# The second keys' grams between the two sums of P, two unread products for three, and the weights rounded in six parts

## The chip, the cores and the metric

The kernel runs on one core of a Trainium2 chip. The metric is the device time of one execution in microseconds (us). TensorE multiplies matrices, VectorE (DVE) and ScalarE (ACT) do elementwise work, GpSimd (POOL) does too, and SyncE (SP) issues most transfers. TensorE's weight loads are listed as an engine of their own (PEld).

## The reference

Three stages in a row. The first is a delta rule over 768 time steps for 4 batches and 8 heads of dimension 48. The second is a linear layer pair with a product. The third is a soft mixture with 8 experts of 4 slots each.

```python
# 1, for every t
y[:, :, t] = einsum('bhd,bhde->bhe', q[:, :, t], state)
v_old = einsum('bhde,bhd->bhe', state, kt)          # kt = k / (|k| + 1e-6)
state = state + bt[:, :, :, None] * einsum('bhd,bhe->bhde', kt, vt - v_old)
# 2, x is y as 3072 tokens of 384
h = (x @ w1) * (x @ w2) @ w3                        # d_ff 1024
x = h @ w_out
# 3, phi is 384 x 32
logits = x @ phi
d = softmax of logits over the tokens; c = softmax over the slots
slot_input = d.T @ x
slot_out[e] = relu(slot_input[e] @ e1[e]) @ e2[e]
out = c @ slot_out
```

## The kernel before

The 768 time steps are cut into 24 tiles of 32 steps (`g` = 0 to 23), 4 tiles to an iteration (`n` = 0 to 5). A tile holds 4 batches times 32 steps in the 128 partitions.

For an iteration the inner products of all keys of a tile with each other and with the queries ("grams", `gram_products`, L1087) are made on TensorE. Out of them a triangular system is solved by elementwise steps (`set_up`, `set_up_rest`, then 30 steps of a product and a sum), scaled (`scale`, L831 and L834) and turned (`turn_back`, L840) into `TM`. For the first iteration VectorE does the 30 steps itself (L819, L820). For each later iteration GpSimd does them (L485, L486), while the tiles of the iteration before are worked on. `scale(n + 1)` on VectorE waits for GpSimd's last step and stands, in VectorE's order, in front of a product a * b of tile `4n + 3` (`ab_mul`, L745).

For each tile TensorE then multiplies keys and queries with the state (`key_query_state`, L1103), solves (`solve_rows`, L1118, which waits for `TM`), updates the state (L1137), makes y (`y_step`, L1152), turns it (`x_turn`, L1164), and multiplies the turned x with w1 and w2 (`up`). Tile 0 does so in plain float32 (L1180). All later tiles use three products of high and low halves (L1201), for which ScalarE rounds the weights to `whi` (`w_high`, L598) and VectorE makes the rest `wlo` (`w_low`, L848). The product a * b is turned by `ab_turn` (L1219).

Ahead of the tiles stands a prologue. P = w3 @ w_out @ phi is made in two steps: w_out with phi (L1273), a sum of its partial results (`add_parts`, L1265), then w3 with that (L1284), and a second sum (L1265). ScalarE copies between them (`part_out`, L602, and the copies to `wp_sb`, L608, and `P_sb`, L614).

Behind the second sum TensorE makes the grams of the second iteration, waits for P, and runs three 128 x 512 products that nobody reads, each after a semaphore (L1299 to L1301). In front of the first grams stand `FILLERS` tiny products (L1255) that nobody reads either. A float32 product is two weight loads and two matmul instructions, so 47 fillers show as x94 and three products as x6.

Every engine runs its list in order. SP issues in this order: first keys, phi, the transposed w_out, the two halves of the transposed w3, the second keys (eight transfers of 192 KB, 1.5 MB), values, w1, w2.

ScalarE's order in the prologue and in tiles 0 and 1 is: first sums, `key_merge` for tile 1, second sums and P, the four pairs of gram copies, `w_high(0)`, Z of tile 0, x of tile 0 (`y_out`), the turned x of tile 0 (`x_high`), `w_high(1)`, then a of tile 0.

## Time and profile before

| what | value |
|---|---|
| three runs | 493.09, 494.03, 495.74 us; median 494.03 |
| the profiled execution | 495.12 us, its span 493.4 us |
| busy share of the span | TensorE 91%, VectorE 50%, ScalarE 46%, GpSimd 38% |
| mean granted TensorE clock | 0.969 of full speed |
| chain of work that ended last | TensorE 71%, VectorE 10%, GpSimd 8%, DMA 5% |

A row of a timeline gives start and duration in us, engine, source line, operation, tiles, shape and count, and in brackets the engine's idle time before it with what ended it. "issue" there means that nothing which the profile shows was waited for. [...]

### The profile page before, as it was taken

The page shows a single profiled execution, that of the slowest core. Times are in us where ns is not written, and L with a number is a line of the kernel's source. Part 1 is how long each engine was busy: PE and PEld are TensorE (multiplying, and loading weights), DVE is VectorE, ACT ScalarE, POOL GpSimd, SP SyncE. Part 2 cuts the span into 40 slices and gives each one's busy share as a digit, 9 for nine tenths or more (in the row PEclk, how much of TensorE's full clock was granted, in tenths as well). Part 3 has the DMA queues.
Part 4 walks back from the last instruction along what each step waited for, and adds up shares of the span by engine and source line. Part 5 has one row for each costly group of instructions (what it writes and reads, how often), then busy time and mean ns, then how long its engine had stood idle before and what let it go on. Part 6 is the DMA issues. An engine that isn't in the chain of part 4 may idle for free.

```text
span 493.4 us, 21402 instructions
## 1 busy us (share of the span) xinstructions
PE 450.5 (91%) x9729; PEld 323.8 (66%) x9729; DVE 244.4 (50%) x499; ACT 227.9 (46%) x408; POOL 188.4 (38%) x329
## 2 busy tenths in 40 slices
PE   4674899998999999999999999999999999999982
PEld 3243467776777777687677777676787777754442
DVE  3899586355553647346284345644362422144123
ACT  1313455553645555655455565554564464224112
POOL 1001499811588403886028880178830000000000
PEclk9965999999999999999999999999999999999997
DMA  8999305320004400054000641000080094699949
GB/s 205 383 243 336 87 3 112 104 49 5 3 19 113 132 5 3 3 131 130 4 3 4 125 116 24 3 4 4 3 337 9 3 356 160 241 418 425 420 169 372
DMA packets 21002, 64.96 MB, mean 132 GB/s; under 512 B 2352, under 2 KB 3760, under 8 KB 20016
## 3 DMA queue, kind: packets, MB, share of 16 engines
q1 hardware_dynamic: 20208, 62.71, 38.7%
q8 instruction: 77, 1.26, 1.1%
q10 hardware_dynamic: 704, 0.89, 0.7%
q14 instruction: 13, 0.11, 0.1%
HBM read 58.87 MB, written 4.72 MB: 129 GB/s over the span
## 4 chain that ended last, share of the span: by engine, by line
PE 71%; DVE 10%; POOL 8%; DMA 5%; issue 3%; SPq 1%; ACT 0%; DVEq 0%; POOLq 0%
PE pA L1201 19%; PE pB L1201 18%; PE pKY L1103 4%; POOL prep_slab L486 4%; DMA step_slab<-e_dram 4%; POOL prod_p L485 4%; PE pD L1137 3%; PE pKY L1152 3%; PE pKY L1118 3%; PE pT L1219 3%; PE pG L1219 3%; PE pD L1227 2%; DVE prep_slab L820 2%; DVE prod_p L819 2%; DMA arena<-kq_dram 2%
## 5 line engine op out<-in xcount | busy, mean ns | idle before, releaser
L485 POOL TENSOR_TENSOR prod_p<-prep_slab 128x30 f32<-128x30 f32 (+9 forms) x150 | 75.4, 502 | 42.4 <-DVE prep_slab L812 31.5
L745 DVE TENSOR_TENSOR arena<-a_sb,pB 128x512 f32<-128x512 f32 x41 | 28.1, 686 | 120.3 <-PE pB L1201 120.2
L486 POOL TENSOR_TENSOR prep_slab<-prep_slab,prod_p 128x30 f32<-128x30 f32 (+9 forms) x150 | 82.4, 549 | 11.8
L524 ACT ACTIVATE step_slab<-pKY 32x384 f32<-32x384 f32 x92 | 44.3, 482 | 32.8 <-PE pKY L1152 31.1
L1201 PE MATMUL pB<-whi,xhi 128*128 128x512 f32 x135 | 55.8, 414 | 0.0
L1201 PE MATMUL pB<-whi,xlo 128*128 128x512 f32 x135 | 53.2, 394 | 0.0
L1201 PE MATMUL pB<-wlo,xhi 128*128 128x512 f32 x135 | 53.2, 394 | 0.0
L1201 PE MATMUL pA<-whi,xhi 128*128 128x512 f32 x135 | 51.4, 436 | 0.0
L1201 PE MATMUL pA<-wlo,xhi 128*128 128x512 f32 x135 | 47.0, 399 | 0.0
L1201 PE MATMUL pA<-whi,xlo 128*128 128x512 f32 x135 | 46.1, 397 | 0.0
L466 POOL TENSOR_TENSOR arena<-arena,nrm 128x1152 f32<-128x1152 f32 (+1 forms) x11 | 21.1, 1914 | 45.7 <-DVE prep_slab L834 45.0
L552 ACT ACTIVATE a_sb<-pA 128x512 f32<-128x512 f32 x47 | 28.1, 598 | 15.7 <-PE pA L1201 14.8
L478 POOL TENSOR_SCALAR_AFFINE_SELECT prep_slab<-prep_slab 128x1024 f32<-128x1024 f32 x5 | 6.3, 1265 | 74.3 <-DVE sys_s L785 74.3
L556 ACT ACTIVATE arena<-pG 128x512 f32<-128x512 f32 x24 | 14.4, 599 | 39.3 <-PE pG L1219 39.3
L516 ACT ACTIVATE step_slab<-pKY 128x768 f32<-128x768 f32 (+1 forms) x24 | 19.2, 799 | 22.3 <-PE pKY L1118 22.3
L1201 PEld LDWEIGHTS pB<-whi,xhi 128*128 128x128 f32 x135 | 25.3, 187 | 6.1
L1201 PEld LDWEIGHTS pB<-whi,xlo 128*128 128x128 f32 x135 | 25.4, 188 | 5.8
L1201 PEld LDWEIGHTS pA<-whi,xlo 128*128 128x128 f32 x135 | 25.4, 188 | 5.6
L556 ACT ACTIVATE arena<-pT 128x512 f32<-128x512 f32 x24 | 14.3, 598 | 31.6 <-PE pT L1219 31.5
L1201 PEld LDWEIGHTS pB<-wlo,xhi 128*128 128x128 f32 x135 | 25.4, 188 | 4.8
L1201 PEld LDWEIGHTS pA<-wlo,xhi 128*128 128x128 f32 x135 | 25.4, 188 | 4.7
L542 ACT ACTIVATE step_slab<-arena 48x512 f32<-48x512 f32 x46 | 26.4, 620 | 0.4
(284 smaller groups left out, 889.1 us busy)
## 6 DMA issues: line engine op xcount, KB each, us to landing
arena<-e_dram SPq DMA_DIRECT2D x7, 1536.0 KB, 14.6
arena<-kq_dram SPq DMA_DIRECT2D x44, 192.0 KB, 5.6
late_w<-e_dram SPq DMA_DIRECT2D x4, 1536.0 KB, 10.7
arena<-kv_dram SPq DMA_DIRECT2D x6, 768.0 KB, 5.2
arena<-kv_dram SPq DMA_DIRECT2D x24, 192.0 KB, 5.9
arena<-w3t_dram SPq DMA_DIRECT2D x2, 2048.0 KB, 19.2
arena<-w_dram SPq DMA_DIRECT2D x1, 4096.0 KB, 13.9
out_dram<-late_w SPq DMA_DIRECT2D x6, 576.0 KB, 5.4
```

Of the source, the lines that this page charges most:

```text
L466: nc.gpsimd.tensor_tensor(v, v, nr, ALU.mult).then_inc(vp_done, 1)
L485: link(nc.gpsimd.tensor_tensor(pv, a, x, ALU.mult))
L486: link(nc.gpsimd.tensor_tensor(dst, dst, pv, ALU.add))
L516: nc.scalar.activation(Z[:, banks], pKY[:, banks, 0:DM], ACT.Copy).then_inc(z_done, 1)
L524: nc.scalar.activation(xs[quad(b), :], pKY[quad(quarter(g, b) ^ 1), bank(g, b), 0:DM], ACT.Copy).then_inc(y_done, 1)
L542: nc.scalar.activation(KM[rows_, :, 1 - x], src[:, :, x], ACT.Copy).then_inc(km_done, 1)
L552: nc.scalar.activation(a_sb[:], up_bank(t, half, 0), ACT.Copy).then_inc(a_done, 1)
L556: nc.scalar.activation(ABT[:, s, half * 4:half * 4 + 4].rearrange("p c t -> p (c t)"), (pT, pG)[half][:], ACT.Copy).then_inc(abt_done, 1)
L745: nc.vector.tensor_tensor(ab_tile(s, p)[:, half * HF:(half + 1) * HF], a_sb[:], up_bank(t, half, 1), ALU.mult).then_inc(ab_done, 1)
L1103: last = mm(pKY[o:o + 64, b % 2, h * D:h * D + D], KM[r:r + D, b // 2 * H + h].rearrange("p x c -> p (x c)"), ST[r:r + D, b // 2, h * D:h ...
L1201: last = mm(up_bank(t, half, w), lhs[:, c * 128:(c + 1) * 128], rhs[:, w, c, fc], start=(k == 0), stop=(k == 3 * KC - 1))
L1219: last = nc.tensor.transpose((pT, pG)[half][:, c * 128:(c + 1) * 128], ab_tile(s, p)[:, f0:f0 + 128], ident[:])
```

## The change

The eight transfers of the second keys are issued ahead of the two halves of w3. On TensorE the grams of the second iteration move from behind the second sum to between the first sum and the wait for its copy; on ScalarE their copies move in front of the second `part_out` pair. One of the three unread products (the one behind the second half of the scaling) is dropped, and one filler is added. `w_high` rounds a third of a weight at a time, and its six calls are spread over tiles 0 and 1; `w_low` waits for three of them.

```diff
-FILLERS = 47
+FILLERS = 48
...
+            reload_kq(1, 1)
             load_w3t(0)
             load_w3t(1)
-            reload_kq(1, 1)
             load_kv(0, 0)
...
-            def w_high(i):
+            def w_high(i, c):
                 act.wait_ge(w12_in[i], 16)
-                nc.scalar.activation(whi[:, i], w_raw[i], ACT.Copy).then_inc(whi_done, 1)
+                nc.scalar.activation(whi[:, i, c], w_raw[i][:, c], ACT.Copy).then_inc(whi_done, 1)
...
+            for i in range(STEPS):
+                gram_out(1, i, first_gram[1][i])
+                pt_copy(1, i)
             part_out(2, 128)
             part_out(3, 128)
             act.wait_ge(p_ps, 1)
             nc.scalar.activation(P_sb[:].rearrange("p a b -> p (a b)"), pY[:, 0:FC * NS], ACT.Copy).then_inc(p_done, 1)
-            for i in range(STEPS):
-                gram_out(1, i, first_gram[1][i])
-                pt_copy(1, i)
-            w_high(0)
...
                         z_out(g)
+                        w_high(0, 0)
                         y_out(g)
+                        w_high(0, 1)
                         continue
...
                     x_high(t)
                     if g == 1:
-                        w_high(1)
+                        w_high(0, 2)
+                        w_high(1, 0)
...
                     a_out(t, 0)
+                    if g == 1:
+                        w_high(1, 1)
+                        w_high(1, 2)
...
-                dve.wait_ge(whi_done, i + 1)
+                dve.wait_ge(whi_done, KC * (i + 1))
...
             add_parts(pK, 32 * KC, wp_ps)
+            pe.wait_ge(gs_done, STEPS)
+            pe.wait_ge(pt_raw, STEPS)
+            for r in range(2):
+                pe.wait_ge(kq_in[1][r], keys_landed(1, 0))
+            apart(pe, pe_passed)
+            for pair in range(2):
+                gram_products(1, pair, first_gram[1][2 * pair:2 * pair + 2])
             pe.wait_ge(wp_done, 1)
...
             add_parts(pY, 128, p_ps)
 
-            pe.wait_ge(gs_done, STEPS)
-            pe.wait_ge(pt_raw, STEPS)
-            for r in range(2):
-                pe.wait_ge(kq_in[1][r], keys_landed(1, 0))
-            apart(pe, pe_passed)
-            for pair in range(2):
-                gram_products(1, pair, first_gram[1][2 * pair:2 * pair + 2])
             pe.wait_ge(p_done, 1)
 
-            for sem_, i in ((r_done, 1), (x_link, 1), (x_link, 2)):
+            for sem_, i in ((r_done, 1), (x_link, 1)):
```

## Rows read from the trace of the kernel before

**Rows 1.** The page's slices: granted TensorE clock in tenths, 40 equal slices

```profile
PEclk9965999999999999999999999999999999999997
```

**Rows 2.** The chain that ended last, in order of time: start us, us, what

```profile
45.89 2.03 DVE TM L840
...
48.40 1.17 DVE prep_slab L777
...
55.19 1.24 DVE prep_slab L812
...
98.94 1.24 DVE prep_slab L831
100.31 0.69 DVE arena L745
101.04 0.66 PE pG L1219 x4
```

**Rows 3.** Timeline of TensorE, prologue, tile 0 and start of tile 4

```profile
16.56 3.19 PE L1273 MATMUL pKY<-arena,phi_sb 128*32 128x512 f32 x12 [3.52 <-DMA arena<-wot_dram]
...
22.96 3.41 PE L1284 MATMUL pKY<-arena,wp_sb 128*32 128x512 f32 x16 [0.47 <-ACT wp_sb L608]
28.61 2.89 PE L1284 MATMUL pKY<-arena,wp_sb 128*32 128x512 f32 x16 [2.24 <-DMA arena<-w3t_dram]
32.20 3.62 PE L1265 MATMUL pKY<-same,TM 128*128 128x32 f32 x16 [0.70 <-ACT TM L602]
...
46.22 4.65 PE L1301 MATMUL pKY<-Macc,ident 128*128 128x512 f32 x6
50.80 0.88 PE L1118 MATMUL pKY<-step_slab,TM 32*32 32x48 f32 x64
...
55.00 2.84 PE L1180 MATMUL pA<-late_w,cN 128*128 128x512 f32 x6 [0.58 <-ACT cN L546]
...
99.80 1.15 PE L1103 MATMUL pKY<-step_slab 48*64 48x48 f32 x64
```

**Rows 4.** Waits, 0 to 120 us: in total, times, longest

```profile
DVE prep_slab L831 <- POOL prep_slab L486: 4.2, 1, 4.2
```

**Rows 5.** Timeline of VectorE, end of the first system

```profile
43.91 0.56 DVE L724 TENSOR_TENSOR step_slab<-arena,nrm 128x384 f32<-128x384 f32 x1
...
45.64 0.22 DVE L834 TENSOR_TENSOR prep_slab<-sys_s 128x32 f32<-128x32 f32 x1
```

**Rows 6.** Waits of TensorE, 33 to 102 us

```profile
PE pB L1087 <- issue: 6.4, 1, 6.4
```

**Rows 7.** Windows: busy us (instructions) by engine, granted clock, DMA share, GB/s

```profile
16.00:24.00 8.00, 6.18 (x36) 3.04 (x40) 7.11 (x28) 2.62 (x4) 0.00 (x0) 0.91 1.05 387
26.00:34.00 8.00, 5.07 (x29) 2.31 (x25) 7.35 (x20) 1.19 (x2) 0.00 (x0) 0.71 1.06 231
...
46.00:49.00 3.00, 3.00 (x24) 1.28 (x9) 3.00 (x3) 2.64 (x5) 2.12 (x1) 0.50 1.04 407
50.00:52.00 2.00, 1.69 (x67) 0.79 (x65) 1.84 (x5) 0.98 (x2) 1.26 (x1) 1.00 1.01 197
```

**Rows 8.** Timeline of ScalarE, tile 0

```profile
47.97 2.76 ACT L598 ACTIVATE whi<-late_w 128x3072 fp32r<-128x3072 f32 x1
51.75 0.49 ACT L516 ACTIVATE step_slab<-pKY 128x384 f32<-128x384 f32 x1 [1.02 <-PE pKY L1118]
53.33 0.49 ACT L521 ACTIVATE step_slab<-pKY 128x384 f32<-128x384 f32 x1 [1.08 <-PE pKY L1152]
54.45 0.49 ACT L546 ACTIVATE cN<-pT 128x384 f32<-128x384 f32 x1 [0.64 <-PE pT L1164]
```

**Rows 9.** Timeline of GpSimd, three neighbouring steps of the second system

```profile
67.14 0.91 POOL L485 TENSOR_TENSOR prod_p<-prep_slab 128x210 f32<-128x210 f32 x1
68.12 2.62 POOL L486 TENSOR_TENSOR prep_slab<-prep_slab,prod_p 128x210 f32<-128x210 f32 x1
70.82 0.59 POOL L485 TENSOR_TENSOR prod_p<-prep_slab 128x220 f32<-128x220 f32 x1
```

## Prediction

> **What bounds the kernel.** I read the page's slices first. TensorE's granted clock is the thing to see there: two early slices at 6 and 5 tenths, full speed from the fifth slice almost to the end [rows 1]. So the only stretch in which TensorE is both idle at times and at the lower level is the first 50 us, which is the stretch the change edits. I then read the chain of work that ended last, in order of time. Up to 101 us it does not run over TensorE. VectorE solves the first set of keys alone, turns it back at 45.89, prepares the second set until 55.19 + 1.24 = 56.4, hands it to GpSimd, takes it back at 98.94 (`scale(1)`), multiplies a * b at 100.31, and only then TensorE's turn of that product starts, at 101.04 [rows 2]. Behind that the chain is TensorE almost throughout.
>
> The next view is TensorE's timeline. Its key and query products of step 4 (L1103) run from 99.80 to 100.95, and its next instruction is the turn at 101.04 (L1219) [rows 3]. VectorE's product ends at 100.31 + 0.69 = 101.00 [rows 2]. So at 101 us the two paths meet within 0.1 us. TensorE, early or late, must pass this meeting point, and VectorE's product stands behind `scale(1)` in its own order, which waits for GpSimd's last step (idle 4.2 us) [rows 4].
>
> **The change part by part.**
> *The products nobody reads.* Before, the second grams end at 46.22, and then three products run to 50.87, 4.65 us or 1.55 us each [rows 3]. The first solve's TM is ready when the turn back ends, at 45.89 + 2.03 = 47.92 [rows 2], yet the solve (L1118) starts at 50.80 [rows 3]. That is 2.9 us of lateness, and these products are its cause. Afterwards the grams are meant to be done earlier, product one may start when L724 is through, 43.91 + 0.56 = 44.47, and product two waits for the first half of the scaling, which ends just before L834 starts at 45.64 [rows 5]. Two at 1.55 us back to back end at 47.57. The solve then starts at the TM, about 48.0: 2.8 us earlier.
>
> *The grams.* They must fit between the two sums. By the rows before: the first product of w3 takes 3.41 us, the second 2.89, the last sum 3.62 [rows 3]. One pass through the grams held a hole of 6.4 us that no semaphore explains ("issue") [rows 6]. I take this for instructions that had not arrived, since DMA was saturated all through it. The next 1.5 MB of keys now go ahead of w3. At 387 and 231 GB/s (DMA of 16 to 24 and of 26 to 34 us [rows 7]) they take 4.1 to 6.8 us, so the second half of w3, in by 28.61 before [rows 3], is in by 32.7 to 35.4. Add 3.41 for its product, 0.7 for the copy and the wait to the sum (the step from the product's end at 31.50 to the sum at 32.20), 3.62 for the sum and 0.5 for ScalarE's copy of P: 40.9 to 43.6, before 44.47. With one hole of 6.4 us inside the grams, and the grams starting when the keys are in (the load in front of them is in at 16.56, when the product that waits for it starts [rows 3], so 20.7 to 23.4, but not before the first sum, which ends shortly before the w3 product at 22.96): 23.4 + 2.5 of grams + 1.3 + 6.4 = 33.6, two products 6.8 make 40.4, the rest 4.8 makes 45.2, then two unread products 3.1, 48.3. Still earlier than 50.80. I take the undisturbed case, 48.0, and keep 48.3 and the two-hole case (below) for the range.
>
> [...]
>
> *The six parts.* ScalarE's rounding of w1 was one piece of 2.76 us for 3072 columns; 384 columns take 0.49 [rows 8]. So a column costs 2.27 / 2688 = 0.84 ns, and a part of 1024 takes 1.03 us. Six make 6.2 us against 5.5, 0.7 us more of an engine busy 46% of the span. The first part fits: between the end of the Z copy (51.75 + 0.49) and the x copy at 53.33 lie 1.09 us. The second does not: from 53.33 + 0.49 = 53.82 to the next copy, 54.45, lie 0.63 us, and TensorE's first large products (L1180, 55.00) wait for that copy [rows 3, 8]. So 0.4 us is given back. Parts three and four (2.1 us) lie beside L1180's first six, 2.84 us [rows 3], and five and six beside the next ones. Without that cover each would cost 1.03 us.
>
> *The rest.* One more filler adds 1 of 48 tiny products in TensorE's wait for the first keys: nothing. It also makes up for the unread product removed, so that all that follows has the same number of TensorE instructions ahead of it. On SP the eight key issues pass two w3 issues; the bytes ahead of values, w1 and w2 are the same. The first keys lie ahead of all of this, and VectorE's chain begins with them: nothing.
>
> **The sum.** TensorE runs 2.8 - 0.4 = 2.4 us earlier from 48 to 98.6 us. Then it arrives at the turn (L1219) and waits, because VectorE's product still ends at 101.0. No part of the chain of [rows 2] is touched: set_up(1) on VectorE follows the turn back and one mask and started at 48.40 in the chain with nothing to wait for, so earlier grams don't hasten it. GpSimd's chain starts at 56.4 as before. So of 2.4 us there remain the 0.1 us that TensorE stood at 101.04. The profiled execution took 495.12 us (span 493.4 and 1.7 around it); less 0.1, 495.0. It lies 1.1 above the median of the three, 494.03, so in terms of the median: 493.9 us.
>
> What can move this is the length of GpSimd's chain, because VectorE's operations now fall on other steps of it. One step took 2.62 us while its twin in size took 0.59 to 0.9 [rows 9], in the stretch where VectorE makes the low halves of the weights. All that VectorE does between 56.4 and 98.9 stays inside, so the number of collisions is the same, but one of four such groups can turn out 2 us dearer or cheaper. I take 0 and allow -1.5 to +2.
>
> **The rivals.** 0.5% or 2.5 us is about what a measurement of this kernel can tell from no change.
> (a) *The 2.4 us get through.* This needs GpSimd's chain 2.4 us shorter, say without the 2.0 us of excess in the one step of [rows 9] and a little more. Price: at most 2.4 us, because then TensorE is the bound: 491.6. Against it: nothing in the change takes work from either engine. 0.10.
> (b) *The sum of P comes late* (the other side). A second hole of 6.4 us, or one longer than that, puts the end of the unread products at 48.3 + 6.4 = 54.7, that is 3.9 us behind 50.80, plus 0.4 at the x copy, less 0.1 of slack: +4.2, 498.2. It decides as soon as the solve starts later than 50.5, because TensorE has only 0.1 us at 101. For it: the grams held the one hole seen, and they now stand in front of P. Against it: a single one is absorbed. 0.14.
> (c) *TensorE stays at the lower clock.* Granted 0.50 in 46 to 49, 1.00 in 50 to 52 [rows 7]: the rise came behind three dense products that followed directly on grams. Now two products follow a pause, and after them only small ones come until 52.6. If the clock is still low there, the 2.84 us of L1180 become up to 5.7; two such groups cost 5.7 us at most, 5.7 - 2.4 - 0.1 = +3.2, 497.1; one costs 2.84 - 2.5 = +0.3, nothing one sees. It decides from 2.5 us of loss on. 0.11.
> [...]
> (d) *My forecast*, the gain swallowed at the meeting point at 101 us: 0.65, with its own range 492.4 to 495.9.
>
> **Numbers.** Faster by over 0.5%: only (a) at its very end, or a mis-sized GpSimd chain: 0.08. Slower by over 0.5%: most of (b), half of (c): 0.16. The rest 0.76. The range leaves out the end of (b): 491.9 to 496.9.
>
> **What would show it.** In the changed kernel: L1301 with two products and L1118 behind them at about 48.0; the hole, if any, inside grams that now lie before 36 us; six roundings of about 1.03 us and the first copy for TensorE's large products 2.4 us earlier; then, as the decisive row, TensorE's turn L1219 still at about 101.0 with some 2.4 us of idle time before it, put down to VectorE's product, and VectorE's wait before L831 still ended by GpSimd near 98.9. I am wrong if that turn starts 1 us or more earlier or later, or if anything behind 101 us differs in length.

## The result: 0.8% slower, and where the time went

The changed kernel takes 499.07 us (median of 7 runs, 497.22 to 499.92) where the kernel before takes 494.73 us (7 runs, 493.09 to 496.73). The ratio is 1.0083, with a 95% interval of 1.0065 to 1.0102. The profiled execution took 499.21 us with a span of 497.5 us, 4.1 us over the span before. The prediction was 493.9 us, in a range that ended at 496.9.

The changed kernel has its own line numbers, 5 more than before in most places: L765 is the first mask that was L760, L836 is `scale` (L831 before), L1224 the turn (L1219), L1123 the solve (L1118), L1092 the gram products (L1087), L1306 the unread products (L1301), L1185 the first large products (L1180).

The chain of work that ended last, in order of time (start, us, what), of the changed kernel:

```profile
3.19 8.47 DMA arena<-kq_dram
11.71 0.33 PE pG L1092 x4
12.87 3.69 issue
16.56 0.33 PE pT L1092
16.91 1.04 DVE prep_slab L765 x2
...
51.71 1.16 DVE prep_slab L782
```

The reader is to see the second and third line. The first keys are in at 11.7, TensorE makes almost all of their grams, and then stands for 3.69 us in front of the last load and pass of one product for pT. Before, the second set-up by VectorE was in this chain at 48.40 [rows 2]; the same operation (L782) is now at 51.71, 3.3 us later.

VectorE's timeline around the first masks, in the kernel before (start, us, line, operation, tiles, and in brackets the idle time ahead):

```profile
12.71 0.59 DVE L760 TENSOR_TENSOR prep_slab<-pG,upto 128x256 f32<-128x256 f32 x1 [7.13 <-PE pA L1087]
...
13.59 0.60 DVE L760 TENSOR_TENSOR prep_slab<-pB,upto 128x256 f32<-128x256 f32 x1
```

And in the changed kernel, with the end of GpSimd's part 85 us later:

```profile
12.56 0.59 DVE L765 TENSOR_TENSOR prep_slab<-pG,upto 128x256 f32<-128x256 f32 x1 [6.99 <-PE pA L1092]
...
16.91 0.59 DVE L765 TENSOR_TENSOR prep_slab<-pB,upto 128x256 f32<-128x256 f32 x1 [3.32 <-PE pT L1092]
...
102.21 1.23 DVE L836 TENSOR_TENSOR prep_slab<-prep_slab,sys_s 128x1024 f32<-128x1024 f32 x1 [4.64 <-POOL prep_slab L486]
...
103.58 0.68 DVE L750 TENSOR_TENSOR arena<-a_sb,pB 128x512 f32<-128x512 f32 x1
```

The third mask starts 3.3 us later, at 16.91 for 13.59. `scale(1)` starts 3.3 us later, at 102.21 for 98.94 [rows 2]. Between the two nothing of the chain VectorE, GpSimd, VectorE has changed its length. Behind them stands the product a * b, and behind that TensorE's turn.

TensorE's timeline of the changed kernel, up to its first large products and at the turn:

```profile
16.56 0.31 PE L1092 MATMUL pT<-arena 48*32 48x64 f32 x1 [3.69 <-issue]
...
32.20 0.33 PE L1092 MATMUL pT<-arena 48*32 48x64 f32 x4 [4.46 <-issue]
...
38.66 0.33 PE L1092 MATMUL pB<-arena 48*32 48x64 f32 x4 [4.43 <-issue]
...
39.27 5.15 PE L1296 MATMUL pKY<-arena,wp_sb 128*32 128x512 f32 x32
45.15 1.97 PE L1270 MATMUL pKY<-same,TM 128*128 128x32 f32 x16 [0.73 <-ACT TM L602]
47.94 2.95 PE L1306 MATMUL pKY<-Macc,ident 128*128 128x512 f32 x4 [0.82 <-DVE step_slab L729]
51.30 1.47 PE L1123 MATMUL pKY<-step_slab,TM 32*32 32x48 f32 x64 [0.42 <-DVE TM L845]
...
56.27 3.96 PE L1185 MATMUL pA<-late_w,cN 128*128 128x512 f32 x5 [0.78 <-ACT cN L546]
...
104.32 0.66 PE L1224 MATMUL pG<-ident,arena 128*128 128x128 f32 x4 [0.56 <-DVE arena L750]
```

Against [rows 3] the reader is to see four things. The new hole of 3.69 us at 16.56 stands where no hole was. The second grams now hold two holes, of 4.46 and 4.43 us, in place of the one of 6.4 us [rows 6]. The sum of P (the second L1270) ends at 47.1, where the prediction had P ready at 40.9 to 43.6, and the solve starts at 51.30, not at 48.0. And the turn starts at 104.32 for 101.04, directly behind VectorE's product. Up to the end of the program TensorE then stays behind by 2.6 to 4.3 us. Of the 4.1 us of the span, 3.3 are there at 101 us. The other 0.8 come in small steps behind that.

Two waits of the changed kernel stand in these rows and are easily overlooked. The first unread product (47.94) waits for L729, and the solve (51.30) for L845, both on VectorE. P was copied by 47.54. So in this kernel the late chain on VectorE, and not the late P, sets the start of the solve.

### The profile page after: what moved, and what is told of

The parts are those of the page before. It is cut to its first block, busy times and chain, and to the rows that moved or that the text cites. A ratio compares the mean times of both kernels' runs of the same rounds, so it can differ in the third digit from the quotient of the medians.

```text
span 497.5 us, 21406 instructions
## 1 busy us (share of the span) xinstructions
PE 450.4 (91%) x9729; PEld 323.0 (65%) x9729; DVE 243.6 (49%) x499; ACT 228.0 (46%) x412; POOL 188.4 (38%) x329
## 3 DMA queue, kind: packets, MB, share of 16 engines
q8 instruction: 77, 1.26, 1.1%
## 4 chain that ended last, share of the span: by engine, by line
PE 70%; DVE 10%; POOL 8%; DMA 5%; issue 4%; SPq 1%; ACT 0%; DVEq 0%; POOLq 0%
PE pA L1206 18%; PE pB L1206 18%; PE pKY L1108 4%; POOL prep_slab L486 4%; POOL prod_p L485 4%; PE pKY L1157 3%; DMA step_slab<-e_dram 3%; PE pD L1142 3%; PE pKY L1123 3%; PE pT L1224 3%; PE pG L1224 3%; PE pD L1232 2%; DVE prep_slab L825 2%; DVE prod_p L824 2%; PE pT L1092 2%
## 5 line engine op out<-in xcount | busy, mean ns | idle before, releaser
L486 POOL TENSOR_TENSOR prep_slab<-prep_slab,prod_p 128x30 f32<-128x30 f32 (+9 forms) x150 | 81.1, 541 | 11.7
L1206 PE MATMUL pA<-wlo,xhi 128*128 128x512 f32 x135 | 47.1, 399 | 0.0
L466 POOL TENSOR_TENSOR arena<-arena,nrm 128x1152 f32<-128x1152 f32 (+1 forms) x11 | 21.9, 1993 | 49.0 <-DVE prep_slab L839 48.3
L556 ACT ACTIVATE arena<-pG 128x512 f32<-128x512 f32 x24 | 14.4, 598 | 40.1 <-PE pG L1224 40.1
L516 ACT ACTIVATE step_slab<-pKY 128x768 f32<-128x768 f32 (+1 forms) x24 | 19.2, 799 | 25.0 <-PE pKY L1123 25.0
L556 ACT ACTIVATE arena<-pT 128x512 f32<-128x512 f32 x24 | 14.4, 598 | 32.0 <-PE pT L1224 31.9
L1092 PE MATMUL pT<-arena 48*32 48x64 f32 x640 | 18.8, 241 | 11.2 <-issue 10.1
## 6 DMA issues: line engine op xcount, KB each, us to landing
arena<-e_dram SPq DMA_DIRECT2D x7, 1536.0 KB, 14.4
```

Of the source, the lines that this page charges most:

```text
L466: nc.gpsimd.tensor_tensor(v, v, nr, ALU.mult).then_inc(vp_done, 1)
L486: link(nc.gpsimd.tensor_tensor(dst, dst, pv, ALU.add))
L516: nc.scalar.activation(Z[:, banks], pKY[:, banks, 0:DM], ACT.Copy).then_inc(z_done, 1)
L556: nc.scalar.activation(ABT[:, s, half * 4:half * 4 + 4].rearrange("p c t -> p (c t)"), (pT, pG)[half][:], ACT.Copy).then_inc(abt_done, 1)
L1092: last = mm(banks[i][quad(quarter(s, b)), h * 64:h * 64 + 64], KQ[p][r:r + D, b // 2, h, 0, C * s:C * s + C], KQ[p][r:r + D, b // 2, h, :, ...
L1206: last = mm(up_bank(t, half, w), lhs[:, c * 128:(c + 1) * 128], rhs[:, w, c, fc], start=(k == 0), stop=(k == 3 * KC - 1))
```

## The experiments

### Only the number of fillers, from both sides

e1_after47 is the changed kernel, and in it only:

```
-FILLERS = 48
+FILLERS = 47
```

> The whole change but with 47 fillers, as before. Theory F (the filler): the 48th filler moved the last product of the first grams past the end of the instructions that were there, so TensorE stood 3.7 us in front of it and VectorE's chain, which sets the time up to 101 us, began 3.3 us late. Then the hole in front of the last first gram is gone, VectorE's third mask (L765) starts near 13.6 again instead of 16.9, and the time is 3.3 us or more below the changed kernel's 499.1: 494.5 to 495.8, no different from before by 0.5%. Theory D (the key transfers ahead of w3 hold up the code): the hole stays, the time stays near 499.

Measured: 494.73 us, ratio to before 0.9986 (0.9968 to 1.0004). So without the 48th filler the whole rest of the change costs and gives nothing that can be measured. TensorE's and VectorE's timelines of this run:

```profile
31.50 0.32 PE L1092 MATMUL pT<-arena 48*32 48x64 f32 x3 [3.13 <-issue]
...
37.97 0.32 PE L1092 MATMUL pB<-arena 48*32 48x64 f32 x3 [4.42 <-issue]
...
48.14 3.39 PE L1306 MATMUL pKY<-Macc,ident 128*128 128x512 f32 x4 [0.47 <-ACT P_sb L617]
51.46 0.88 PE L1123 MATMUL pKY<-step_slab,TM 32*32 32x48 f32 x64
```

```profile
14.39 0.59 DVE L765 TENSOR_TENSOR prep_slab<-pB,upto 128x256 f32<-128x256 f32 x1
...
99.78 1.23 DVE L836 TENSOR_TENSOR prep_slab<-prep_slab,sys_s 128x1024 f32<-128x1024 f32 x1 [4.48 <-POOL prep_slab L486]
```

The hole in the first grams is gone, the two in the second grams are not. `scale(1)` is 0.8 us later than before because the first keys landed 0.8 us later in this execution (the first mask ran at 13.52, for 12.71).

e2_before48 is the kernel before, and in it only the opposite edit:

```
-FILLERS = 47
+FILLERS = 48
```

> The kernel before with one filler more and nothing else. Theory F: a hole of about 3 to 4 us in front of the last product of the first grams, everything on VectorE 3.3 us later, 498.0 (3.3 above before). Theory D: no hole, no difference from before.

Measured: 497.96 us, ratio 1.0054 (1.0036 to 1.0072). TensorE's and VectorE's timelines:

```profile
16.69 0.31 PE L1087 MATMUL pT<-arena 48*32 48x64 f32 x1 [3.86 <-issue]
```

```profile
17.04 0.59 DVE L760 TENSOR_TENSOR prep_slab<-pB,upto 128x256 f32<-128x256 f32 x1 [3.50 <-PE pT L1087]
...
102.33 1.23 DVE L831 TENSOR_TENSOR prep_slab<-prep_slab,sys_s 128x1024 f32<-128x1024 f32 x1 [5.47 <-POOL prep_slab L486]
```

The same hole, in a kernel that has nothing else of the change. One tiny product that nobody reads makes `scale(1)` 3.4 us later. By the ratios the filler costs 0.5% here, and 1.0% between e1_after47 and the changed kernel (0.9986 and 1.0083). The traces show 3.3 to 3.4 us in VectorE's chain in both, which is 0.7%, and the intervals leave room for that in both.

### Why one filler: counting TensorE's instructions

Each filler is four instructions in the trace, two weight loads and two passes, and the first grams are 512. I counted TensorE's loads and passes from the start of each trace up to every hole of over 1 us that is put down to "issue":

```
kernel          fillers   first grams end at no.   "issue" holes stand behind no.
before            47            700                1209
changed           48            704                702, 954, 1210
e1_after47        47            700                954, 1210
e2_before48       48            704                702, 1209
e3_keys_first     47            700                1209, 1463
e4_after111      111            956                446, 702, 957, 1210, 1466
e5_after31        31            636                446, 954, 1209
e10_before_two    47            700                1209, 1463
```

The places are the same in every kernel to within 3, and 252 to 256 apart, whatever stands there. The small differences come from the count, which leaves out TensorE's semaphore instructions and drains, of which the trace records 349 (347 and 2). With them all such holes ahead of 60 us, in all 18 kernels, stand behind 449, 705, 961, 1217 or 1473, exactly 256 apart, and so it goes on to the end: the largest "issue" waits of the kernel before behind 105 us (at 110.5, 116.1, 310.9 and 409.5 us) stand behind 4289, 4545, 14017 and 18369, all of them 449 plus a multiple of 256. The page of the changed kernel has a DMA queue for instructions. These are its rows for TensorE and for that queue:

```profile
PE 450.4 (91%) x9729; PEld 323.0 (65%) x9729; DVE 243.6 (49%) x499; ACT 228.0 (46%) x412; POOL 188.4 (38%) x329
...
q8 instruction: 77, 1.26, 1.1%
```

It moved 77 packets in 1.26 MB, 16.4 KB each. TensorE's 9729 passes and as many loads are 19,458 instructions, with the 349 others 19,807, or 77.4 pieces of 256. e4_after111 (below) has 256 more loads and passes and 78 packets. And in all 18 kernels each hole of over 1 us ahead of 60 us, 38 of them, ends 1.2 to 1.6 us behind the end of a packet on q8. So in these traces TensorE's instructions come in pieces of 256 through the DMA engines. Such a piece is what is late. The first grams end at number 700 with 47 fillers, two short of the end of a piece. With 48 they end at 704, and the last load and pass of the last product, which VectorE's third mask waits for, stand in the next piece. In the kernel before, the same piece came no earlier than it was needed either (its packet ended at 14.4 us, behind the end of the grams at 12.9), but TensorE was waiting for `wot` there until 16.56 [rows 3]. The DMA view of the changed kernel between 12 and 18 us shows what the piece had to share the engines with:

```profile
q1 hardware_dynamic: 590, 1.67, 101.7%
...
q8 instruction: 1, 0.02, 1.1%
```

One packet of instructions beside 590 of data, which fill all 16 engines. By its record that packet ended at 15.0 us, and instruction 703 started at 16.56. Of the 38 holes 37 stand in stretches with a DMA share of 1.01 to 1.10 and are 1.40 to 7.29 us long; the last, of 1.69 us at 57.10 in e3_keys_first, has 0.42. There are such waits without DMA too: those of the kernel before at 116.1 and 310.9 us, 1.24 and 1.23 us long, have a share of 0.00. And a full share is not needed for a long one: e7_after31_short has one of 3.06 us at 372.16 with 0.39.

### More and fewer fillers

My guess, for which no trace has a record, was that the next piece is asked for when TensorE gets into the present one. Then many more fillers should have pulled every piece ahead, and far fewer should only have shifted things. e4_after111 and e5_after31 are the changed kernel with

```
-FILLERS = 48
+FILLERS = 111
```

> The whole change with 111 fillers: 64 more than 47, that is 256 more TensorE instructions, all run in the idle time before the first keys land at 5.2. Theory F in its stronger form (code comes in pieces of 256 instructions, and each piece is asked for when the piece before the last is used up): the boundaries fall at the same products as with 47, but each piece is asked for earlier, so the hole in the first grams is gone and the holes of 4.5 and 4.4 us in the second grams shrink or go; time 494.5 to 495.5. If a filler costs because of its own time, this is slower than with 48: over 499.

Measured: 499.77 us, ratio 1.0086 (1.0061 to 1.0111). TensorE's timeline:

```profile
10.66 0.33 PE L1092 MATMUL pG<-arena 48*32 48x64 f32 x4 [4.64 <-issue]
...
17.13 0.33 PE L1092 MATMUL pG<-arena 48*32 48x64 f32 x4 [4.44 <-issue]
```

My theory that earlier requests close the holes was wrong: there are now five, of 3.3 to 7.3 us, two of them in the first grams, because the ends of pieces (446 and 702) lie inside them and TensorE reaches 446 before its piece has landed (5.8 us, for a packet that ended at 9.1).

```
-FILLERS = 48
+FILLERS = 31
```

> The whole change with 31 fillers: 64 TensorE instructions fewer than with 47. Theory M (pieces of 256 instructions, and up to 101 us the time is set by the chain VectorE, GpSimd, VectorE alone): with 47 the second grams held two holes, 3.1 and 4.4 us, because two boundaries fell into them; now one boundary falls just in front of them and one just behind, so one hole remains, the first unread product starts at L729 (about 44.5 to 45.5) instead of 48.1, the solve 2 to 3 us earlier than 51.5, and the time is still that of 47 fillers, 494.7, within 1.5 us, because TensorE waits at the turn near 101. Theory T (TensorE sets the time): 2 to 3 us faster than with 47, about 492.

Measured: 500.90 us, ratio 1.0118 (1.0092 to 1.0145), the slowest kernel of all. Its first grams end at 636, far from 702, and yet:

```profile
13.77 0.33 PE L1092 MATMUL pB<-arena 48*32 48x64 f32 x4 [2.48 <-issue]
```

That hole is the end of the piece at 446. With 45 to 48 fillers the piece behind 446 landed at 7.6 to 8.9 us, in all kernels. Here it ended at 12.4. TensorE, which runs its fillers while it waits for the first keys, had got to number 124 when they came, for 180 and more in the others; that this is why the piece came late is my reading, and e4_after111 (9.1 us) shows that still more fillers don't bring it earlier. So the fillers seem to do two things: they pull the piece behind 446 ahead, and they put the end of the grams at a number. 47 serves both, 31 only the second, 48 only the first. That is not all of the 31 fillers' cost. In this trace `scale(1)` is 2.4 us late, but TensorE is 5.3 us late at 101 us by its own path (the solve starts at 53.38), and 9.4 at 450 us; the profiled execution (504.38 us) was also the slowest of the five.

### The order of the transfers alone

e3_keys_first is the kernel before, and in it only:

```
             sp.dma_start(wot_raw, ...)
+            reload_kq(1, 1)
             load_w3t(0)
             load_w3t(1)
-            reload_kq(1, 1)
```

> The kernel before with only the order of the transfers changed (second keys ahead of w3), 47 fillers. Theory F: no hole in the first grams. The sum of P ends some us later, but three unread products still end near 51 to 54, so 0 to +3 us against before. Theory D: a hole of 3 to 4 us in the first grams and +3.3 us.

Measured: 500.61 us, ratio 1.0088 (1.0060 to 1.0115). TensorE's, then VectorE's timeline:

```profile
30.55 3.64 PE L1284 MATMUL pKY<-arena,wp_sb 128*32 128x512 f32 x16 [5.42 <-DMA arena<-w3t_dram]
...
50.31 4.47 PE L1301 MATMUL pKY<-Macc,ident 128*128 128x512 f32 x6
```

```profile
102.64 1.23 DVE L831 TENSOR_TENSOR prep_slab<-prep_slab,sys_s 128x1024 f32<-128x1024 f32 x1 [0.58 <-POOL prep_slab L486]
```

With the keys in front and the grams left behind the sum of P, w3's second half comes 7.2 us later than in [rows 3] (its product starts at 35.83 for 28.61), TensorE waits for both halves, and the grams start late. The unread products run from 50.31 instead of 46.22, and the second set-up on VectorE waits for the grams (it starts at 51.76). So the new order alone costs 4 to 5 us, and e1_after47 shows that the rest of the change with 47 fillers pays it back, and no more. That it is the moved grams that do so, and not the dropped product or the six parts, is likely but was not tried alone.

### What the first chain is worth: a shorter first system

e6_before_short is the kernel before with a narrower update in the first solution. It leaves out all but the first column in steps 13 to 18 of the first solution:

```
-    pv, a, x, dst = update(prod_p, X, k_, 0, k_)
+    pv, a, x, dst = update(prod_p, X, k_, 0, 1 if 13 <= k_ < 19 else k_)
```

> The kernel before, with six of the thirty steps of the first system (13 to 18) narrowed to one column on VectorE: it leaves out part of that solution and saves VectorE some 2.5 us; the counts of instructions and waits stay. Theory M: VectorE has its first TM 2.5 us earlier, but the second grams (46.2, held up by their 6.4 us hole) and the three unread products (50.9) stay where they are. So TensorE is as late as before and the time falls by 0.1 to 0.5 us only: 494.5 to 495.3. If the chain alone set the time whatever TensorE does: 2.5 us less, 492.9.

Measured: 494.26 us, ratio 0.9988 (0.9969 to 1.0006). VectorE's timeline:

```profile
42.75 0.56 DVE L724 TENSOR_TENSOR step_slab<-arena,nrm 128x384 f32<-128x384 f32 x1 [2.05 <-DMA arena<-kv_dram]
```

VectorE got through sooner and then waited 2.05 us for the first values. Only 0.8 us of chain was left (`scale(1)` at 98.11), and 0.5 of it were there from the start (the third mask at 13.10 for 13.59). The run says nothing of TensorE, but it shows the next floor: the landing of the values at 42.75.

e7_after31_short is e5_after31 with the same narrowing, so it leaves out the same part.

> The changed kernel with 31 fillers and the same six steps narrowed (part of the first solution left out). Theory M: now grams and P are ready early enough, so the chain of VectorE and GpSimd and TensorE's solve both move, and the time is 1.5 to 2.5 us below the same kernel without the narrowing, about 492.5. That is then what the change is worth: it makes room that the first system must use. If nothing is gained here either, TensorE or P is the bound before 101 us.

Measured: 498.79 us, ratio 1.0080 (1.0052 to 1.0107), 2.1 us under e5_after31. Its `scale(1)` ran at 98.54, earlier than in the kernel before, and still it is slower by 0.8%. At 101 us its TensorE is 0.4 us ahead of the kernel before, at 300 us 0.8 behind and at 450 us 6.5 behind. So the whole loss of this execution, the slowest of its six, lies in TensorE's later work. Behind 105 us it stood 8.4 us for "issue", against 6.3 before; the rest of the loss is open.

### Six parts or two

e8_after47_whole is e1_after47 with the weights rounded in two whole pieces, the first ahead of the Z copy and the second behind x:

```
+                        w_high(0)
                         z_out(g)
-                        w_high(0, 0)
                         y_out(g)
-                        w_high(0, 1)
...
-                        w_high(0, 2)
-                        w_high(1, 0)
+                        w_high(1)
...
-                        w_high(1, 1)
-                        w_high(1, 2)
```

> The changed kernel with 47 fillers and the weights rounded in two pieces as before, the first ahead of Z of tile 0, the second behind the turned x. Theory M: TensorE's first large products (L1185) start some 0.4 us earlier relative to y of tile 0, and the time stays within 0.5 us of the 47-filler kernel, because the turn near 101 waits for VectorE all the same. If ScalarE's rounding mattered: at least 0.4 us of difference in either direction beyond the interval.

Measured: 495.01 us, ratio 1.0003 (0.9985 to 1.0021), no difference from e1_after47 that can be told. Here TensorE's solve did start early, at 49.39, and the turn then waited. The waits of TensorE up to 110 us:

```profile
PE pG L1219 <- DVE arena L745: 1.1, 1, 1.1
```

TensorE did not bring the 1.4 us of the solve to the turn. Its first six large products took 4.40 us for 2.84, at a mean granted clock of 0.64, so it reached the turn at 100.62, 0.3 us ahead of the kernel before. There it waited 1.1 us, because `scale(1)` was 0.7 us late (99.60), as the first keys were 0.6. The early solve itself comes from the two unread products, which took 1.98 us here, at a granted clock of 1.00, and 3.39 in e1_after47, at 0.58, and from a P that was ready 0.7 us sooner.

### The unread products

e9_after47_none is e1_after47 without any unread products:

```
-            for sem_, i in ((r_done, 1), (x_link, 1)):
-                pe.wait_ge(sem_, i)
-                mm(pK[:], ident[:], Macc[:, 0:HF], start=True, stop=True)
```

> The changed kernel with 47 fillers and none of the unread products. With 47 fillers they ran from 48.1 to 51.5 and held the first solve back behind the TM of 48.7. Theory M (TensorE must wait at the turn near 101 for VectorE): the solve starts up to 2.8 us earlier and the turn does not; the time stays at 494.7 plus or minus 1, or rises if the clock stays at the lower level through the first large products. Theory T (TensorE sets the time): 2 to 3 us faster, 492.

Measured: 492.87 us, ratio 0.9962 (0.9946 to 0.9979), faster than both kernels. TensorE's timeline, and the windows of 48 to 52 and 52 to 58 us (the seventh figure is the granted clock, as a share of full speed):

```profile
47.77 1.24 PE L1123 MATMUL pKY<-step_slab,TM 32*32 32x48 f32 x64 [1.63 <-DVE TM L845]
...
53.27 5.36 PE L1185 MATMUL pA<-late_w,cN 128*128 128x512 f32 x6 [0.58 <-ACT cN L546]
```

```profile
48.00:52.00 4.00, 2.72 (x127) 2.38 (x114) 3.73 (x10) 2.31 (x4) 1.27 (x1) 0.52 1.04 325
52.00:58.00 6.00, 5.42 (x9) 2.13 (x8) 3.86 (x13) 3.06 (x4) 1.30 (x5) 0.50 0.39 92
```

The solve starts 3.0 us earlier than in [rows 3], ended by VectorE's TM as the prediction had it. But the granted clock stays at 0.52 and 0.50 in these two windows, and the first six large products take 5.36 us where they took 2.84 [rows 3]. At 58 us TensorE is 0.8 us later than before, not earlier. So the gain of this kernel does not come from this stretch. It appears in small steps behind 101 us (0.8 us at 114, 1.8 at 296).

e10_before_two takes one unread product away from the kernel before, and nothing else:

```
-            for sem_, i in ((r_done, 1), (x_link, 1), (x_link, 2)):
+            for sem_, i in ((r_done, 1), (x_link, 1)):
```

> The kernel before with two unread products instead of three and nothing else. Theory M: the solve 1.5 us earlier, the wait of the turn near 101 longer by as much, time within 0.5 us of before. Theory T: 1.5 us faster, 493.

Measured: 496.33 us, ratio 1.0033 (1.0013 to 1.0054). TensorE's timeline:

```profile
52.25 0.44 PE L1118 MATMUL pKY<-step_slab,TM 32*32 32x48 f32 x19 [1.40 <-issue]
...
55.97 4.54 PE L1180 MATMUL pA<-late_w,cN 128*128 128x512 f32 x6 [0.58 <-ACT cN L546]
```

TensorE stands 1.40 us in the middle of the solve, at the end of the piece behind 1463. That end lies inside the solve with three products too (the solve is 128 loads and passes long and begins behind number 1376 then, behind 1372 here), and e3_keys_first, with three, has the same hole at 57.10. What differs is when TensorE gets there. In the kernel before it came at 51.26, 1.5 us behind the landing of the piece (49.77); here at 50.65, and the piece landed at 50.87, 1.1 us later than before. How much of that the missing product did, and how much this one execution, is open. Then the large products run at a mean granted clock of 0.62, 4.54 us for 2.84, and TensorE arrives at the turn 2.1 us late.

The low clock does not follow the number of unread products alone. With three of them one of six traces shows the first large products slow (4.32 us for 2.84 at a mean granted clock of 0.65, e3_keys_first), with two four of eight (4.40 to 4.54 at 0.62 to 0.64), with none or two tiny ones three of four (4.98 to 5.36 at 0.52 to 0.57); in the other ten they took 2.84 us at 1.00. The fewer, the more often, but no number decides it.

### Taking work from GpSimd

If the meeting point at 101 us holds a gain back, a shorter GpSimd chain should let it through. In e11_after47_none_taken VectorE makes the last 8 of GpSimd's 30 steps, inside `scale`, on top of e9_after47_none:

```
+TAKEN = 8
...
-                for k_ in range(1, C - 1):
+                for k_ in range(1, C - 1 - TAKEN):
...
+                    for k_ in range(C - 1 - TAKEN, C - 1):
+                        pv, a, x, dst = update(prod_p, X, k_, 0, k_)
+                        link(nc.vector.tensor_tensor(pv, a, x, ALU.mult))
+                        link(nc.vector.tensor_tensor(dst, dst, pv, ALU.add))
```

> The changed kernel with 47 fillers, no unread products, and the last 8 of GpSimd's 30 steps of each system done by VectorE, which stands idle for GpSimd at that place. GpSimd's last 8 steps took 7.6 us in the trace of before, VectorE's own same steps 5.0 us. Theory M: both paths to the turn near 101 now come earlier, the chain by 2.6 us, TensorE by up to 2.8, so 1.5 to 2.6 us faster than the same kernel without the taken steps: 492 to 493. Theory T says the steps do nothing.

Measured: 496.89 us, ratio 1.0031 (1.0008 to 1.0054). The profiled execution (494.68 us) was the fastest of the twelve. In it `scale(1)` ran at 97.51, 1.4 us earlier, and the granted clock was 1.00 from 48 to 58 us this time, with the large products at 2.84 us from 52.42. TensorE was 1.4 us ahead at 105 us, and all but 0.1 of it was gone by 370 us. The waits of TensorE over the whole run show one reason, 6 turns instead of 1:

```profile
PE pG L1232 <- DVE arena L753: 4.6, 6, 0.8
```

e12_before_taken is the same edit on the kernel before.

> The kernel before with the same 8 steps taken by VectorE. The scaling before the turn near 101 comes 2.6 us earlier, but TensorE arrives there at 100.95 as before: 0.1 us from there, and up to 0.5 where a later turn waited for VectorE. Theory M: 0.1 to 0.6 us faster, not to be told from before. If the chain alone set the time: 2.6 us faster.

Measured: 498.73 us, ratio 1.0063 (1.0036 to 1.0089). `scale(1)` came 1.8 us later, at 100.76, and the turns again waited 4.6 us in 6. GpSimd's shorter part ended at 91.96, but VectorE began its eight steps at 95.78, behind a product a * b that waited for TensorE, so the chain now hung on TensorE as well. In each of the five solutions that GpSimd makes, VectorE's own steps now stand in front of a * b, and the turn waits 0.8 us. In the four behind the first that is 3.2 us, more than the edit gives at 101. It is the one cost that the traces name; the medians, above those of the same kernels without the edit by 4.0 and 3.9 us, ask for more.

The forecasts for e3_keys_first, e5_after31, e7_after31_short, e10_before_two, e11_after47_none_taken and e12_before_taken all missed on the slow side. The time of e9_after47_none is near what "TensorE sets the time" forecast, but its trace does not bear that out: at 101 us TensorE was 0.2 us late.

### Is the later gain a matter of the count too?

Without the unread products eight instructions are gone from the count of all that follows. Four kernels were to separate that from the products' own time. e13_after47_two_tiny puts two tiny products in place of the two unread ones in e9_after47_none:

```
+            for sem_, i in ((r_done, 1), (x_link, 1)):
+                pe.wait_ge(sem_, i)
+                mm(pK[0:32, 0:32], ident[0:32, 0:32], ident[0:32, 0:32], start=True, stop=True)
```

> The kernel without unread products was 0.4% faster than before, and behind 105 us TensorE's 'issue' waits were 4.0 us in all, for 6.3 before. Theory (the count): removing two products takes 8 instructions (two products of two passes, each with its load) out of the count of all that follows, so that later ends of pieces fall at cheaper places. Here two products of 32 columns stand in their place and restore the count. By the count: the gain is gone, ratio 0.998 to 1.000, about 494.5 us, 'issue' waits behind 105 us near 5. Rival (the products' own time): they only had to be short, and the gain stays, ratio 0.996, 493 us.

Measured: 494.50 us, ratio 0.9976 (0.9960 to 0.9991).

e14_after45 is the changed kernel with `FILLERS = 45`.

> The changed kernel with 45 fillers: from the first grams on, the count is the one of the kernel without unread products, but the two unread products stay. By the count: as fast as that one, ratio 0.996, 493 us. By the rival: like 47 fillers, 0.9986, 494.7 us. Both: no hole in the first grams, which end at number 692.

Measured: 494.19 us, ratio 0.9964 (0.9946 to 0.9982).

e15_before46 is the kernel before with `FILLERS = 46`.

> The kernel before with 46 fillers: the first grams end at number 696, inside the piece, and all that follows moves by four instructions towards the start. Both theories: no hole in the first grams. By the count, if four instructions matter: a time off the one before by up to 0.3% either way; by the rival: the same time, ratio 1.000.

Measured: 494.67 us, ratio 0.9986 (0.9966 to 1.0005).

e16_after45_none is e9_after47_none with `FILLERS = 45`.

> No unread products and 45 fillers: 8 instructions further towards the start. If the later gain comes from where the ends of pieces fall, it changes again, by 0.5 to 2 us either way, with the 'issue' waits behind 105 us; by the rival it stays at 0.996, 492.9 us.

Measured: 492.93 us, ratio 0.9950 (0.9932 to 0.9968), the lowest ratio of the study, but by the time no different from e9_after47_none (492.87). All four ran beside the same runs of before (495.75 us).

The forecasts by the count came nearer than the rival's for e13_after47_two_tiny, whose interval just reaches the rival's 0.996, and for e14_after45, whose interval leaves out the rival's 0.9986. The other two did not decide. e15_before46 could lie up to 0.3% off by the count and not at all by the rival, and its interval holds 1.000. e16_after45_none was to change by 0.5 to 2 us by the count and to stay by the rival; it moved by 0.1 us in time and by 0.6 us in the ratio.

TensorE's waits for "issue" behind 105 us, added up over one profiled execution each:

```
kernel                 us in all   ratio to before
before                 6.3         1
e1_after47             5.1         0.9986
e13_after47_two_tiny   5.1         0.9976
e15_before46           4.4         0.9986
e8_after47_whole       4.2         1.0003
e14_after45            4.1         0.9964
e9_after47_none        4.0         0.9962
e16_after45_none       3.6         0.9950
```

In this table the three fastest have the smallest sums, and e14_after45, which has the count of e9_after47_none and the products' time, reaches the same ratio. That speaks for the count. But the intervals overlap, and e8_after47_whole, e15_before46 and the forecast for e16_after45_none don't follow, and kernels left out of the table have small sums without being fast, for other reasons (e4_after111 3.0, e11_after47_none_taken 3.6). The changed kernel itself has 6.0 us here, so its own 0.8 us behind 101 are not explained by this sum. That the later gain comes from the count is supported, not shown, and the 0.8 us stay open.

e14_after45 gave something else. Its TensorE timeline at the solve, the first large products and the turn:

```profile
47.71 0.88 PE L1123 MATMUL pKY<-step_slab,TM 32*32 32x48 f32 x64 [0.32 <-DVE TM L845]
...
52.09 2.84 PE L1185 MATMUL pA<-late_w,cN 128*128 128x512 f32 x6 [0.78 <-ACT cN L546]
...
100.71 0.66 PE L1224 MATMUL pG<-ident,arena 128*128 128x128 f32 x4 [3.14 <-DVE arena L750]
```

In this execution the keys landed early (first mask at 12.44), the two holes in the second grams took 2.8 and 4.1 us, P was ready in time, and the large products had a granted clock of 1.00 (48 to 58 us). These are the rows that the prediction forecast: the solve 3.1 us earlier at the TM, and then 3.14 us of idle time ahead of the turn, which starts only 0.3 us earlier than before. Two things are not as forecast. The kernel is 0.36% faster by its ratio, some 1.8 us, where 0.1 was forecast. And the idle time may have a price. Behind it the granted clock was 0.50, as the window of 102 to 104 us shows, in which the kernel before had 1.00:

```profile
102.00:104.00 2.00, 2.00 (x61) 1.25 (x64) 1.85 (x2) 1.06 (x1) 0.34 (x1) 0.50 0.04 8
```

TensorE came to the turn 3.4 us ahead of the kernel before, left it 0.3 us ahead, is 1.0 us behind it at 105 us, and level with it at 114 us. So in this execution the gain that was swallowed at the meeting point turned into a small loss just behind it.

## Why the prediction was wrong, point by point

**The step that failed** is the sentence "One more filler adds 1 of 48 tiny products in TensorE's wait for the first keys: nothing", and with it "The first keys lie ahead of all of this, and VectorE's chain begins with them: nothing". The filler's own time is covered by the wait for the keys, and that was right. The prediction also counted, but only for what stands behind the removed product, where one filler more and one product less make the same number. Everything between the two, the first grams above all, moves by four instructions, and it did not ask what that does. The end of the first grams moved from number 700 to 704, over the end of a piece at 702, and that put 3.3 us into the chain of VectorE and GpSimd, which I had left untouched. Shown by e2_before48 (the filler alone: ratio 1.0054) and e1_after47 (all but the filler: 0.9986). I had read the hole of [rows 6] as instructions that had not arrived, which was right, and had then reckoned with it only inside the second grams. That DMA was saturated all through that hole holds (a share of 1.02 from 38.5 to 45 us), but it is no condition: behind 105 us the same trace has such waits of up to 1.24 us with a DMA share of 0.00.

**The sum of P undisturbed** failed as well, and beside the filler it cost nothing that shows. I chose no hole (40.9 to 43.6), kept one (48.3), and gave two only to rival (b). The 2.5 and 1.3 us for the grams in that sum have no row beside them; without their hole the grams took 4.1 us before (35.75 to 46.22, less 6.4). The count would have told that two ends of pieces, 954 and 1210, lie in the second grams. They cost 4.46 and 4.43 us in the changed kernel, 3.13 and 4.42 in e1_after47, and P is done near 47.5 and 48.1. The solve started at 51.30 and 51.46, the first held by VectorE's late TM, the second by P and the two unread products behind it. So the 2.8 us that were to be swallowed at 101 were not there to begin with in these two. They were where the unread products took 1.98 us at a granted clock of 1.00 (e8_after47_whole, 1.4 us, and e14_after45, 3.1 us, the latter with P ready before 45.4) or were missing or tiny (2.6 to 3.0 us in e9_after47_none, e13_after47_two_tiny and e16_after45_none, and there a granted clock of 0.50 from 52 to 58 us took them back by 58 us).

**The meeting point at 101 us** held, and e14_after45 shows it with 3.14 us of waiting for a solve 3.1 us earlier. In the changed kernel it worked in the direction that I had not priced: the chain over GpSimd is 3.3 us late, and so TensorE is 3.3 us late. The idle time ahead of the turn, which I had named as the decisive row with 2.4 us, was 0.56.

**Rival (b)** described a late P and forecast 498.2. The time is near, the cause is another: with the late P and 47 fillers the kernel is as fast as before.

**Rival (c)**, the low clock, did happen in the changed kernel (0.64 over the first six large products, 4.39 us for 2.84), whose clock row of the page and window of 56 to 58 us are

```profile
PEclk9957799999999999999999999999999999999998
```

```profile
56.00:58.00 2.00, 1.73 (x2) 0.84 (x3) 1.76 (x9) 2.00 (x3) 0.00 (x0) 0.50 0.14 48
```

against full speed from the fifth slice before [rows 1]. At 58 us TensorE is 2.8 us late, but GpSimd's chain is 3.3 us late, so the latter decides. The clock costs nothing that can be seen beside it.

The first slices of [rows 1] are not to be read as full speed. The trace has no record of the clock ahead of 19.2 us in the kernel before (40.0 in e14_after45), and the profile shows such time as full speed (1.00 for 0 to 12 us). The passes tell otherwise. A pass of the first grams took 0.311 us, as between 35 and 46 us with 0.50 granted, for 0.216 behind 101 us with 1.00. So the first grams ran at the low level. The prediction's sums don't use the start of that row.

**Six parts at 1.03 us**: right in size. ScalarE's timeline of the changed kernel:

```profile
53.34 1.06 ACT L598 ACTIVATE whi<-late_w 128x1024 fp32r<-128x1024 f32 x1
54.40 0.49 ACT L521 ACTIVATE step_slab<-pKY 128x384 f32<-128x384 f32 x1
54.79 1.05 ACT L598 ACTIVATE whi<-late_w 128x1024 fp32r<-128x1024 f32 x1
55.74 0.48 ACT L546 ACTIVATE cN<-pT 128x384 f32<-128x384 f32 x1
```

The copies of x and cN stand back to back with the parts, and the first large product waits 0.78 us for cN, for 0.58 before [rows 3]. So 0.2 us was given back, not 0.4, and e8_after47_whole, without the parts, is no faster.

**GpSimd's chain** was given -1.5 to +2 us for other collisions. It kept its length. That VectorE's work makes a step longer was my estimate; what the traces show is that the one long step of [rows 9] lies beside VectorE's low halves (68.40 to 70.28 us there, 71.61 to 73.49 here), and that it came again:

```profile
71.34 2.61 POOL L486 TENSOR_TENSOR prep_slab<-prep_slab,prod_p 128x210 f32<-128x210 f32 x1
```

## What to carry to other kernels

An instruction that costs nothing by its duration still moves every one behind it in its engine's count. Where a small product releases another engine's long chain, find the "issue" holes in the trace, count the instructions up to them, the semaphore instructions too, and see which product each end of a piece falls on; then price an added or removed instruction by that. Here an end of a piece cost up to 1.24 us in the kernel before with a DMA share of 0.00, and up to 7.3 us in this study with 1.05.

Products nobody reads move when TensorE gets to the next end of a piece and with which instruction (in the kernel before the solve began behind number 1376 with three and 1372 with two, and TensorE got to the end behind 1463 at 51.26 and 50.65 us). And in these traces the clock behind them was low the more often the fewer they were: one of six traces with three, four of eight with two, three of four with none or tiny ones. Take one away only with both rows in view, and try none as well as one fewer: here one fewer gave 1.0033 on the kernel before, and none, with the other edits and 47 or 45 fillers, 0.9962 and 0.9950.

## What was not expected of the hardware

In the traces of this case TensorE's instructions arrive in pieces of 256 (16.4 KB a packet on queue q8, 77 packets for 19,807 instructions), semaphore instructions counted. With a DMA share of 1.01 to 1.10 TensorE stood 1.4 to 7.3 us at such an end, counting holes of over 1 us ahead of 60 us (one of the 38, of 1.69 us, had 0.42), and up to 1.24 us in the kernel before with a share of 0.00. In all 38 of those holes the next instruction started 1.2 to 1.6 us behind the end of the packet's record. When a piece is asked for is not recorded. The landing of one and the same piece, behind number 446, lay between 7.6 and 9.1 us with 45 fillers or more, and at 12.4 and 12.7 us in the two kernels with 31.

Where the trace has no record of the granted clock, ahead of 19.2 us in the kernel before, the page shows full speed. The duration of a pass of known form (0.311 us at 0.50 and 0.216 at 1.00 for the grams) tells the level there: 0.311 us in the first grams.
